# Attention and two feed-forward blocks on one core: four chunks of 2, 3, 3 and 4 tiles in place of three of 4

## What is computed

```python
keep = is_sink | in_window                    # key < 4, or 0 <= query - key < 128
scores = np.where(keep, scale * q @ k.T, -1e9)
a = np.exp(scores - scores.max(-1)); a = a / (a.sum(-1) + 1e-09)
x = a @ v                                     # heads side by side: (1536, 512)
h = x @ w_in
x = (h * (1.0 / (1.0 + np.exp(-1.702 * h)))) @ w_out
gate = 1.0 / (1.0 + np.exp(-(x @ w_gate)))
return (gate * (x @ w_val)) @ w_out2
```

## Time and profile before

| | |
|---|---|
| Median of 3 runs | 717.68 us (717.19 to 719.29) |
| Profiled execution: its time | 715.4 us |
| Profiled execution: span from first to last instruction | 713.6 us |
| TensorE, weight loads | busy 687.4 us (96%), 562.0 us (79%) |
| ScalarE, GpSimd, VectorE | busy 397.4, 354.7, 278.1 us (56, 50, 39%) |
| Granted TensorE clock, mean | 0.997 |
| Transfers | 73.41 MB, 103 GB/s on average |

### The profile page before, as it was taken

The page is one execution under the profiler, slowest core; times in us unless marked ns, Lnnn a source line. Parts: engine busy times, 40 slices in busy tenths (PEclk is TensorE's granted clock), DMA queues, the critical chain, the costliest instruction groups (busy, mean ns, idle before and its releaser), DMA issues.

```text
span 713.6 us, 10667 instructions
## 1 busy us (share of the span) xinstructions
PE 687.4 (96%) x3632; PEld 562.0 (79%) x3632; DVE 278.1 (39%) x820; ACT 397.4 (56%) x855; POOL 354.7 (50%) x419
## 2 busy tenths in 40 slices
PE   6777999999999999999999999999999999999998
PEld 5556788888788888788888788888878888788886
DVE  6888434344444333343443433333232222311112
ACT  4787466667665666466676666565444444433321
POOL 2574245555455545266565655464335445544530
PEclk9999999999999999999999999999999999999999
DMA  6322332343433223143325323311132233233001
GB/s 199 137 75 75 114 113 100 101 144 126 141 116 108 89 73 104 60 148 129 99 98 177 125 82 134 119 60 36 60 141 90 91 126 138 103 110 114 0 1 59
DMA packets 23798, 73.41 MB, mean 103 GB/s; under 512 B 3616, under 2 KB 3616, under 8 KB 23744
## 3 DMA queue, kind: packets, MB, share of 16 engines
q1 hardware_dynamic: 23744, 72.73, 30.9%
HBM read 69.57 MB, written 3.15 MB: 102 GB/s over the span
## 4 chain that ended last, share of the span: by engine, by line
PE 88%; ACT 4%; DVE 3%; issue 2%; SPq 1%; DMA 0%; ACTq 0%; DVEq 0%
PE ps L781 22%; PE ps L782 21%; PE ps L783 21%; PE ps L847 5%; PE ps L848 5%; PE ps L849 5%; PE ps L768 1%; PE ps L766 1%; PE ps L767 1%; PE ps L751 1%; PE ps L738 1%; PE ps L752 1%; PE ps L739 1%; ACT probs L434 1%; DVE probs_n L605 1%
## 5 line engine op out<-in xcount | busy, mean ns | idle before, releaser
L379 POOL TENSOR_TENSOR w_lo<-w_raw,w_hi 128x256 fp32r<-128x256 f32 (+1 forms) x336 | 277.4, 857 | 270.7 <-ACT w_hi L428 270.7
L781 PE MATMUL ps<-x_hi,w_hi 128*128 128x512 f32 x480 | 195.6, 407 | 1.2 <-issue 0.9
L782 PE MATMUL ps<-x_lo,w_hi 128*128 128x512 f32 x480 | 188.2, 392 | 0.0
L783 PE MATMUL ps<-x_hi,w_lo 128*128 128x512 f32 x480 | 187.6, 391 | 0.0
L428 ACT ACTIVATE w_hi<-w_raw 128x1024 fp32r<-128x1024 f32 (+1 forms) x84 | 104.3, 1242 | 42.5 <-PE ps L849 25.9
L621 DVE SCALAR_TENSOR_TENSOR ps<-squashed,ps 128x512 f32<-128x512 f32 x84 | 58.2, 692 | 151.2 <-PE ps L783 88.5
L452 ACT ACTIVATE g_hi<-ps 128x512 fp32r<-128x512 f32 x84 | 50.1, 597 | 110.9 <-DVE ps L621 110.9
L783 PEld LDWEIGHTS ps<-x_hi,w_lo 128*128 128x128 f32 x480 | 90.2, 188 | 20.0
L781 PEld LDWEIGHTS ps<-x_hi,w_hi 128*128 128x128 f32 x480 | 90.2, 188 | 15.8 <-issue 1.7
L782 PEld LDWEIGHTS ps<-x_lo,w_hi 128*128 128x128 f32 x480 | 90.6, 189 | 12.8
L626 DVE TENSOR_TENSOR g_lo<-ps,g_hi 128x512 fp32r<-128x512 f32 x84 | 58.0, 691 | 49.5 <-ACT g_hi L452 49.3
(11 more groups left out here) (75 smaller groups left out, 1006.3 us busy)
## 6 DMA issues: line engine op xcount, KB each, us to landing
w_raw<-in_w SPq DMA_DIRECT2D x36, 768.0 KB, 4.3
w_raw<-in_w SPq DMA_DIRECT2D x48, 512.0 KB, 3.3
q_raw<-in_q_t SPq DMA_DIRECT2D x48, 128.0 KB, 3.7
k_raw<-in_k_t SPq DMA_DIRECT2D x48, 128.0 KB, 3.6
v_raw<-in_v_t SPq DMA_DIRECT2D x12, 256.0 KB, 3.7
out_x<-out_sb SPq DMA_DIRECT2D x12, 256.0 KB, 2.2
v_sink_raw<-in_v_sink SPq DMA_DIRECT2D x2, 160.0 KB, 2.9
k_sink_raw<-in_k_sink SPq DMA_DIRECT2D x4, 8.0 KB, 2.2
```

The costliest lines, as they stand in the source:

```text
L379: pool.tensor_tensor(w_lo[:, slot, at:at + part], w_raw[:, slot, at:at + part], w_hi[:, slot, at:at + part].bitcast(F32), ALU.subtract).th ...
L781: pe.matmul(ps[:, bank, :], hi, act_hi, start=first, stop=False)
L782: pe.matmul(ps[:, bank, :], hi, act_lo, start=False, stop=False)
L783: return pe.matmul(ps[:, bank, :], lo, act_hi, start=False, stop=last)
```

## The change

Four chunks of 2, 3, 3 and 4 tiles (`CHUNK_TILES`) take the place of three of 4. Widths of products, copies and gates follow the chunk: 256, 384, 384 and 512 columns. The counts in semaphore waits follow too. The early stage now has the first chunk's 16 units in 21 slots, with the three early weight splits at slots 6, 11 and 16; beside the chunks run 24, 24 and 32 units. `slot_base` is replaced by `placed`, which counts in columns: the slots of a chunk are spread evenly, 2451, 3716 and 2842 columns apart, with a hole around `LAST_UP`, and a slot's parts follow at multiples of 512 columns, each at the first quantum that starts there or later. Scores stand at 0; transposes of the unit before and the weighing at 1; splits of the transposed probabilities at 2; guard, inverse and normalising at 3, with the `x` parts. In chunk 0 the low parts of keys and queries from the second group on are made by VectorE, after the inverse, and no longer by GpSimd.

```diff
+PART = 512
-OFF_SCORE, OFF_WEIGH, OFF_NORMALISE, OFF_TRANSPOSE = 0, 1, 2, 3
-OFF_SPLIT, OFF_X, OFF_PT = 1, 2, 4
+OFF_SCORE, OFF_TRANSPOSE, OFF_WEIGH, OFF_NORMALISE = 0, 1, 1, 3
+OFF_SPLIT, OFF_PT, OFF_X = 1, 2, 3
+PARTS = 4
...
-def slot_base(n):
-    return 8 * n if n < HOLE else 127 + (n - HOLE) * 59 // 8
...
+def placed(c):
+
+    starts = [0]
+    for r in range(PER_CHUNK):
+        for columns in quanta_in_step(c, r):
+            starts.append(starts[-1] + columns)
+    first_end = starts[first_quantum(c, LAST_UP)]
+    second_start = starts[first_quantum(c, LAST_UP) + 2 * KT - 1]
+    second_end = starts[first_quantum(c, PER_CHUNK - 1)]
+    slots = units_beside(c) + W_LAG
+    spacing = (first_end + second_end - second_start - PARTS * PART) // slots
+    before_hole = (first_end - (PARTS - 1) * PART) // spacing + 1
+    parts = {}
+    for n in range(slots):
+        base = n * spacing if n < before_hole else second_start + (n - before_hole) * spacing
+        for off in range(PARTS):
+            at = next(q for q in range(len(starts)) if starts[q] >= base + off * PART)
+            parts.setdefault(at, []).append((off, n))
+    return parts
...
-EARLY_WEIGHTS = (11, 15, 19)
+EARLY_WEIGHTS = (6, 11, 16)
...
         def tokens(c):
-            return slice(CH * c, CH * c + CH)
+            return slice(P * FIRST_TILE[c], P * FIRST_TILE[c + 1])
...
-                                if u % GROUP == 0:
+                                if u % GROUP == 0 and c > 0:
                                     qk_low_parts(u // GROUP + 1)
...
+            def qk_low_parts(hh):
+                t, half = divmod(hh, 2)
+                heads = slice(half * GROUP, half * GROUP + GROUP)
+                own = slice(t % 2 * P, t % 2 * P + P)
+                dve.wait_ge(qk_high, 2 * (hh + 1))
+
+                dve.wait_ge(qk_low, 2 * hh)
+                dve.tensor_tensor(k_lo[:, heads, own], k_raw[:, heads, :], k_hi[:, heads, own].bitcast(F32), ALU.subtract).then_inc(qk_low, 1)
+                dve.tensor_tensor(q_hl[D:P, heads, :], q_raw[D:P, heads, :], q_hl[D:P, heads, :].bitcast(F32), ALU.subtract).then_inc(qk_low, 1)
...
+                        if c == 0 and u >= EARLY_UNITS + GROUP and u % GROUP == 0:
+                            qk_low_parts(u // GROUP + 1)
...
-                    pe.wait_ge(masked, u + 1 if u % CHUNK_UNITS == CHUNK_UNITS - 1 else u + 2)
+                    if u + 1 in (H * t for t in FIRST_TILE):
+
+                        pe.wait_ge(pt_ready, u)
+                    else:
+                        pe.wait_ge(masked, u + 2)
```

More of the change, by code:

```diff
@@ L1 @@
 from contextlib import ExitStack
+from functools import lru_cache
 import numpy as np
@@ L22 @@
 CH = 512
-NCH = B * S // CH
+CHUNK_TILES = (2, 3, 3, 4)
+NCH = len(CHUNK_TILES)
+FIRST_TILE = tuple(sum(CHUNK_TILES[:c]) for c in range(NCH + 1))
 F1, F2 = 2048 // P, 1536 // P
@@ L72, in parts_at @@
 def parts_at(c, q):
-    if c == NCH - 1:
-        return []
-    return [(off, n) for n in range(CHUNK_UNITS + W_LAG) for off in range(8) if slot_base(n) + off == q]
+    return placed(c).get(q, []) if c < NCH - 1 else []
 class Flow:
@@ L161, in build @@
         ST_BANK, O_BANK = 6, 7
-        early = Flow(CHUNK_UNITS, 2, 3, 4, 5, [5, 0], [6, 1], [O_BANK, 2], fillers=2)
+        early = Flow(EARLY_UNITS, 2, 3, 4, 5, [5, 0], [6, 1], [O_BANK, 2], fillers=2)
         IDLE_BANK = 3
@@ L250, in tokens, with width, copied_before, stores_before @@
         def tokens(c):
-            return slice(CH * c, CH * c + CH)
+            return slice(P * FIRST_TILE[c], P * FIRST_TILE[c + 1])
+        def width(step):
+            return columns_in(step // PER_CHUNK)
+        def copied_before(c, parity):
+            return sum((n + 1 - parity) // 2 for n in CHUNK_TILES[:c])
+        def stores_before(c, tt):
+            return sum(n > tt for n in CHUNK_TILES[:c])
         @block.sync
@@ L294, in _ @@
                 load_weights(step)
-            for t in range(2, 5):
+            for t in range(2, CHUNK_TILES[0] + 1):
                 load_qk(2 * t)
@@ L541, in _ @@
                         if r < LAST_UP or r == PER_CHUNK - 1:
-                            if j == KT + 2 and step + 1 < STEPS:
+                            if j == min(KT + 2, quanta_of(c, r) - 1) and step + 1 < STEPS:
                                 g_high(step + 1)
@@ L619, in gate @@
                 dve.wait_ge(hidden_done, step + 1)
-                bank = gated_bank(step % PER_CHUNK)
-                dve.scalar_tensor_tensor(ps[:, bank, :], squashed[:, step % 2, :], 1.0, ps[:, bank, :], ALU.add, ALU.mult).then_inc(gate_done, 1)
+                bank, n = gated_bank(step % PER_CHUNK), width(step)
+                dve.scalar_tensor_tensor(ps[:, bank, 0:n], squashed[:, step % 2, 0:n], 1.0, ps[:, bank, 0:n], ALU.add, ALU.mult).then_inc(gate_done, 1)
             def g_low(step):
-                slot = step % 2
+                slot, n = step % 2, width(step)
                 dve.wait_ge(g_hi_done, step + 1)
-                dve.tensor_tensor(g_lo[:, slot, :], ps[:, gated_bank(step % PER_CHUNK), :], g_hi[:, slot, :].bitcast(F32),
+                dve.tensor_tensor(g_lo[:, slot, 0:n], ps[:, gated_bank(step % PER_CHUNK), 0:n], g_hi[:, slot, 0:n].bitcast(F32),
                                   ALU.subtract).then_inc(g_ready, 1)
@@ L777, in weigh, with product @@
                     last.then_inc(group_summed, 1)
[L779 removed]
+            def product(to, w_at, act_hi, act_lo, first, last):
                 hi, lo = w_at(w_hi), w_at(w_lo)
[L781 to L783 removed]
+                pe.matmul(to, hi, act_hi, start=first, stop=False)
+                pe.matmul(to, hi, act_lo, start=False, stop=False)
+                return pe.matmul(to, lo, act_hi, start=False, stop=last)
             def from_x(bank, step, at, k):
                 columns = tokens(step // PER_CHUNK)
[L787 removed]
+                return product(ps[:, bank, 0:width(step)], lambda w: w[:, step % RING, at + k * P:at + k * P + P],
                                x_hi[:, k, columns], x_lo[:, k, columns], k == 0, k == KT - 1)
@@ L828, in down1 @@
                 if m == 0 and r == 0 and c > 0:
-                    pe.wait_ge(even_copied, 2 * c)
-                    pe.wait_ge(odd_copied, 2 * c)
-                last = product(Y_BANKS[m], lambda w: w[:, step % RING, DM + m * P:DM + m * P + P],
-                               g_hi[:, step % 2, :], g_lo[:, step % 2, :], r == 0, r == LAST_UP)
+                    pe.wait_ge(even_copied, copied_before(c, 0))
+                    pe.wait_ge(odd_copied, copied_before(c, 1))
+                n = width(step)
+                last = product(ps[:, Y_BANKS[m], 0:n], lambda w: w[:, step % RING, DM + m * P:DM + m * P + P],
+                               g_hi[:, step % 2, 0:n], g_lo[:, step % 2, 0:n], r == 0, r == LAST_UP)
                 if r == LAST_UP:
```

128 lines of the change are left out of this document (68 added, 60 removed).

## The result

| | before | after |
|---|---|---|
| Median of 4 runs each, on the same chip | 717.88 us | 776.50 us (775.33 to 777.32) |
| Ratio, 95% interval | | 1.0813 [1.0789, 1.0836] |
| Profiled execution: time and span | 715.4, 713.6 us | 777.1, 775.1 us |
| Granted TensorE clock, mean | 0.997 | 0.978 |

The account below looks back on a forecast made before the run. VectorE and ScalarE's chain was taken to bound the early stage, TensorE's stream the rest. 715.4 - 33.2 + 16.6 + 6.7 + 11.7 + 1.3 + 4 = 722.5, as a median 725 us; 8 in 10 range 712 to 736.

Parts of the forecast that it names:

- Part 1: Early stage: sixteen units leave it, saving 33.2 us; the moved early weight splits cost nothing.
- Rival (e): Early stage: it does not shrink by 33 us because fewer loads ahead start the next tiles late; chance 0.02.
- Parts 2 and 3: Steady stage on TensorE: sixteen units return beside the chunks, +16.6 us; 672 more, shorter products, +6.7 us (0 to 9).
- part 2: Steady stage: sixteen units come back beside the chunks at 1.04 us of TensorE each, +16.6 us.
- Part 4: Steady stage: transposes sharing bank 6 with scores wait until VectorE has masked them, +11.7 us, from 0 to 20.
- rival (a): Mask waits as short as an idle VectorE allows, 8 us, nothing late behind the queues: 717 us; chance 0.18.
- (b): Mask waits cost next to nothing because TensorE reaches the transposes late anyway: 709 us, up to 713; chance 0.20.
- Parts 5 and 6: One more chunk boundary, +1.3 us; work behind VectorE's pairs and ScalarE's key and query copies, +4 us (0 to 12).
- rival (d): Chunk 0: VectorE's key and query pairs collide with GpSimd's instructions, 5 x 1.5 us, giving 731 us; chance 0.05.
- part 6: Chunk 0 queues: VectorE's key and query pairs 2 us, ScalarE's key and query copies 2 us; together +4, bounds 0 and +12.
- Rival (c): ScalarE becomes the bound in chunk 0's first 16 steps, over 90% busy, +8 us, giving 733 us; chance 0.10.

Follow-up runs that it names:

- e1: The changed kernel with the order within a slot of the kernel before, in the new chunks: 792.4 us, 1.104 of the kernel before.
- e4: The changed kernel with transposes one part later (at 2) and splits of the transposed at 3, in all chunks: 783.5 us, 1.0908 of the kernel before.
- e7: The changed kernel with four chunks of 3 tiles, transposes at 2 and splits of the transposed at 3: 729.6 us, 1.0173 of the kernel before.
- e15: The changed kernel with transposes at 2 and splits of the transposed at 3 in its second chunk alone: 766.3 us, 1.0684 of the kernel before.
- e3: The changed kernel with chunk 0's key and query subtractions back on GpSimd: 765.9 us, 1.067 of the kernel before.
- e12: The changed kernel with, in chunk 0, an own bank for transposes, later transposes and splits, and VectorE normalising instead of ScalarE: 764.0 us, 1.0656 of the kernel before.
- e5: The changed kernel with a PSUM bank of their own for chunk 0's transposes: 763.6 us, 1.0633 of the kernel before.
- e9: The changed kernel with, in chunk 0 alone, an own bank for transposes, transposes at 2 and their splits at 3: 764.7 us, 1.0654 of the kernel before.
- e14: The changed kernel with, in chunk 0, own bank, later transposes, VectorE normalising, and key and query pairs on GpSimd: 754.5 us, 1.0513 of the kernel before.
- e16: The 754.5 us kernel (chunk 0: own bank, later transposes, VectorE normalising, pairs on GpSimd) with chunk 1's transposes at 2, splits at 3: 745.3 us, 1.0394.
- e6: The changed kernel with four chunks of 3 tiles and the new places (transposes at 1): 758.4 us, 1.0584 of the kernel before.

## Why the prediction was wrong, point by point

The profiled executions differ by 777.1 - 715.4 = +61.7 us, their spans by 61.5. Of these the early stage gives -29.9 and the steady stage (from the first score beside the chunks to the end) +91.4.

| term | predicted | measured |
|---|---|---|
| 1 early stage | -33.2 | -29.9 |
| 2 sixteen units beside the chunks | +16.6 | about +17, a remainder |
| 3 more, shorter products | +6.7 | +7.8 |
| 4 transposes that wait for the mask | +11.7, up to +20 | +45.4: 7.4 behind punctual masks, 37.2 behind late ones, the rest ahead of transposes that wait for no mask |
| scores that wait for `pt_lo` | not there | +8.6 |
| 5 boundary, 6 other waits of products | +1.3, part of +4 | +2.5 |
| half clock after waits | not there | about +10 |

**Part 1** was nearly right. The pace of 8.31 us held, but 3.0 us were lost before 28.2 us. The prediction put the early weight splits at nothing from periods later in the stage, and had 3 x 1.06 us for the case without that cover. About 2 of the 3 us come with the first split; no run leaves it out, so that it is the cause is likely, not shown. Rival (e), late loads, can have no more than these 3.3 us.

**Parts 2 and 3.** By the spacings, 672 x 0.120 + 1344 x 0.1725 + 672 x 0.2267 - 2016 x 0.2267 = +7.8 us, within the bounds. The fixed part of a product is 0.120 us less 256 columns at 2.4 GHz, 13 ns. What the Trainium skill gives for it (TensorE: Matmul & The Clock Gate, "Wait — 56ns, not 53.3ns?": about 2.5 ns) doesn't hold here either at 256 columns. Of the 91.4 us of the steady stage, 91.4 - 7.8 - 45.4 - 8.6 - 2.5 = 27.1 are left for the units and the clock. The five stretches shown last 23.7 us at half the clock, which is 11.9 us of TensorE's work, some 1.2 of it while it waited anyway. About 10 us for the clock leave 17 for the units, near the 16.6 of part 2. That is a remainder, but 13.5 us of it can be counted: the usual spacings behind the scores, transposes and weighings are 65.7 us for 80 units, against 52.2 before for 64.

**Part 4 is the step that failed.** Its mechanism was right, and named: the transposes do wait for `neg_max` L637, and mostly behind `g_low` or the gate. Its size came from a model of where TensorE would be. Three of four masks were to find VectorE idle, some 0.2 us each, 8 us in all (rival (a)); the measured 7.4 us behind 43 punctual masks confirm that part. The rest of the term was 11 late masks at 0.2 to 0.6 us. There were 34, at 1.1 us on average and up to 2.9. The model moved the mask behind a gate's chain that runs undelayed; in the run the chain itself is late. In the worst wait the gate stands behind a pair; in the waits at 248.35 and 466.19 us the Tanh or `g_hi` stands behind ScalarE's normalising of the same slot. `g_lo` is late with it, and the mask behind `g_lo`. While VectorE's queue stands there, its low busy share (41% before, 40% now) tells nothing of how late a mask is. So what failed is the number and the size of the late masks: 37 us where the term had some 4.

The upper end was 44 us, 77 waits of at most 0.57 us, halved to 20 without a row that allowed it. That the measured sum is 45 is luck: 24 waits were longer than the "worst", and 43 cost 0.17 us on average. Nor would the full 44 have been enough. With it the range would have ended near 757, and the kernel took 776.5, since two terms were missing.

**What was missing altogether** is the half clock after waits, about 10 us, and the other half of the cycle, 8.6 us here. Scores and transposes share bank 6, so a slot's room must hold two chains one after the other: scores, mask, transposes; and transposes, `pt_hi`, `pt_lo`, next scores. The prediction counted only the first. In chunk 0's 4.8 parts of 0.7 us, the mask has one part (0.7 us) and `pt_lo` 2.8 (2.0 us) with the new places; with the later ones 2 and 1.8. Neither fits, and e1 and e4 show that what is given to the one is taken from the other, and more. With 7.3 parts (e7, chunk 1 in e15) both fit nearly. In the changed kernel the second half costs little; it is what stands in the way of the obvious repair. Rivals (a) and (b) fell by the late masks: (a)'s 8 us are what the punctual masks alone cost, and (b) had less than that.

**Parts 5 and 6, rival (d).** The pairs on VectorE cost 10.6 us (e3), where part 6 had 2 and rival (d) 6 more. A pair without a GpSimd instruction beside it takes what was forecast, one with GpSimd's splits beside it more (VectorE's timeline, two of the five pairs; for the third see the worst wait):

```profile
82.30 0.69 DVE L631 TENSOR_TENSOR k_lo<-k_raw,k_hi 128x512 fp32r<-128x512 f32 x1
83.03 0.69 DVE L632 TENSOR_TENSOR q_hl<-q_raw,q_hl 64x512 fp32r<-64x512 f32 x1
...
158.56 0.77 DVE L631 TENSOR_TENSOR k_lo<-k_raw,k_hi 128x512 fp32r<-128x512 f32 x1
159.36 1.38 DVE L632 TENSOR_TENSOR q_hl<-q_raw,q_hl 64x512 fp32r<-64x512 f32 x1
```

In the worst wait they take 0.98 and 1.10 us, and GpSimd's four splits in the same stretch 3.24 us where four of the mean in the earlier trace rows take 2.96. So rival (d)'s collision exists. The Trainium skill (SBUF — State Buffer, "Who interferes with whom") says that a VectorE instruction with two SBUF inputs contends with a GpSimd instruction that reads SBUF, and these rows agree. But it makes the five pairs only 1.8 us longer in sum. What e3 gives back is mainly 4.8 us ahead of the transposes and 13.6 us less time at half the clock, worth up to 6.8 us; that is (d)'s condition but not its arithmetic.

**Rival (c)**, ScalarE as the bound, is out for its part: ScalarE is busy 65% beside chunk 0 and not 90, and moving the normalising from it to VectorE gained nothing (e12).

**What stays open.** In chunk 0 some 17 us of waits stay even with a bank of their own (e5, e9) and two thirds of that without the pairs as well (e14, e16: 11 to 12 us ahead of the weighing). They sit in the queues of VectorE and ScalarE, and which instruction would have to move was not tried; that chunk 0 is simply too dense for the two, theory C for 256 columns, is not excluded. Nor was a version without half clock stretches made, so the 10 us rest on the records and not on a run.

## What to carry to other kernels

If two uses of a PSUM bank alternate, a slot must hold both chains, each with the queues in which it stands; where it doesn't, moving one instruction only moved the wait here, and more room helped (29 us in e7 against e6), another bank in part (13 us in e5). How late an instruction is in an in-order queue is told by what stands directly ahead of it and whom that waits for, not by the engine's busy share. And a chain timed where nothing is late gives the least that a wait behind it costs, not the most.
